# Token tiles' products of one head each, 64 rows by 96 columns, instead of pairs padded with zeros

## The reference

```python
kv = np.einsum('bhsd,bhse->bhde', k, v)          # 8 batches, 8 heads, 576 tokens, 64 dims
out = np.einsum('bhsd,bhde->bhse', q, kv)
rms = np.sqrt(np.mean(out * out, axis=-1, keepdims=True) + 1e-06)
x = out / rms * g_norm                           # to 4608 tokens of 512
logits = x @ phi                                 # 512 x 32 slots
d = softmax of logits over all tokens;  slot_input = d.T @ x
for e in range(8):                               # 4 slots each
    slot_out[e] = np.maximum(slot_input[e] @ w1[e], 0) @ w2[e]   # 512 x 1024, 1024 x 512
c = softmax of logits over slots;  result = c @ slot_out
```

## Time and profile before

| | us |
|---|---|
| median of 3 runs | 171.68 (171.58 to 171.88) |
| the profiled execution | 171.48 |
| its span, first to last instruction | 170.2 |
| TensorE matmuls busy | 148.9 (88%), 1704 records |
| TensorE weight loads busy | 101.0 (59%), 1704 records |
| ScalarE busy | 88.7 (52%) |
| VectorE busy | 87.4 (51%) |
| GpSimd busy | 59.4 (35%) |
| moved by DMA | 71.63 MB in 3555 packets, 421 GB/s |

### The profile page before, as it was taken

One profiled execution on the slowest core, in us unless ns is written; L12 is line 12 of the kernel. 1 busy time (PEld: TensorE's weight loads), 2 busy tenths in 40 slices (PEclk: granted clock), 3 DMA queues, 4 the chain that ended last, 5 costly groups with the idle time before them and its releaser, 6 DMA issues.

```text
span 170.2 us, 3974 instructions
## 1 busy us (share of the span) xinstructions
PE 148.9 (88%) x1704; PEld 101.0 (59%) x1704; DVE 87.4 (51%) x187; ACT 88.7 (52%) x230; POOL 59.4 (35%) x73
## 2 busy tenths in 40 slices
PE   7989889889999899999998999989999789989200
PEld 3468768789688888787985774333436443454000
DVE  1122607672677265765276799634987037218300
ACT  3036758776965887887498882203233045218300
POOL 7000706767256755385716689200000004000000
PEclk9999999999999999999999999999999999999855
DMA  5999999999999999999999899999799999999997
GB/s 184 422 450 421 432 425 478 420 427 470 442 411 409 459 429 431 474 394 446 455 413 485 351 455 434 412 409 485 332 424 443 431 466 383 421 409 439 415 445 306
DMA packets 3555, 71.63 MB, mean 421 GB/s; under 512 B 746, under 2 KB 746, under 8 KB 881
## 3 DMA queue, kind: packets, MB, share of 16 engines
q1 hardware_dynamic: 3137, 71.20, 97.9%
q0 software_dynamic: 400, 0.18, 0.4%
HBM read 61.94 MB, written 9.44 MB: 419 GB/s over the span
## 4 chain that ended last, share of the span: by engine, by line
PE 53%; DMA 24%; ACT 12%; DVE 3%; issue 1%; SPq 1%
PE psum L93 53%; DMA arena<-in_w_dram 14%; DMA arena<-in_kv_dram 9%; ACT bd L93 3%; ACT arena L93 3%; ACT sq L93 2%; ACT part L93 1%; ACT r L93 1%; SPq L93 1%; DVE ms L93 1%; ACT d L93 1%; DVE logits L93 1%; DVE d L93 0%; DVE part L93 0%; DVE arena L93 0%
## 5 line engine op out<-in xcount | busy, mean ns | idle before, releaser
L93 PE MATMUL psum<-bd,arena 128*128 128x192 f32 (+1 forms) x320 | 55.5, 335 | 3.6 <-ACT bd L93 1.4
L93 PEld LDWEIGHTS psum<-bd,arena 128*128 128x128 f32 (+1 forms) x320 | 45.4, 179 | 10.0 <-ACT arena L93 2.8
L93 PE MATMUL psum<-arena 128*64 128x64 f32 (+2 forms) x896 | 36.2, 270 | 1.1 <-DMA arena<-in_w_dram 0.9
L93 PEld LDWEIGHTS psum<-arena 128*64 128x64 f32 (+2 forms) x896 | 27.5, 129 | 13.4 <-issue 5.2
L93 POOL TENSOR_TENSOR part<-part,r 128x512 f32<-128x512 f32 x17 | 17.8, 1048 | 48.8 <-DVE r L93 48.8
L93 POOL TENSOR_TENSOR arena<-arena,r 128x512 f32<-128x512 f32 x34 | 34.7, 1043 | 0.0
L93 ACT COPY arena<-psum 128x512 f32<-128x512 f32 (+2 forms) x48 | 30.7, 649 | 6.0 <-PE psum L93 5.9
L93 DVE TENSOR_REDUCE ms<-sq 128x16 f32<-128x1024 f32 (+1 forms) x19 | 22.1, 1163 | 22.1 <-ACT sq L93 21.6
L93 ACT ACTIVATE sq<-psum 128x512 f32<-128x512 f32 x36 | 21.5, 596 | 10.9 <-PE psum L93 10.6
L93 ACT COPY part<-psum 128x256 f32<-128x256 f32 (+1 forms) x38 | 13.6, 358 | 12.6 <-DVE part L93 11.5
L93 DVE TENSOR_REDUCE logits<-part 128x64 f32<-128x512 f32 (+1 forms) x18 | 17.8, 990 | 0.1
(11 more groups left out here) (77 smaller groups left out, 110.0 us busy)
## 6 DMA issues: line engine op xcount, KB each, us to landing
arena<-in_w_dram SPq DMA_DIRECT2D x2, 8064.0 KB, 29.1
arena<-in_t_dram SPq DMA_DIRECT2D x1, 6912.0 KB, 36.9
arena<-in_w_dram SPq DMA_DIRECT2D x1, 6400.0 KB, 21.6
arena<-in_w_dram SPq DMA_DIRECT2D x3, 2048.0 KB, 17.9
arena<-in_kv_dram SPq DMA_DIRECT2D x2, 2304.0 KB, 19.7
arena<-in_kv_dram SPq DMA_DIRECT2D x1, 4608.0 KB, 42.2
arena<-in_w_dram SPq DMA_DIRECT2D x1, 4096.0 KB, 24.5
arena<-in_kv_dram SPq DMA_DIRECT2D x1, 3584.0 KB, 31.8
```

The costliest lines, as they stand in the source:

```text
L93: self.inst, self.token = method(*args, **kwargs), None
```

## The change

A pair's matmul over 128 rows and 192 columns becomes two matmuls, one for each head, over that head's 64 rows and 96 columns (32 logit columns and 64 of the output). The rows of a head are the half of the partitions on which its dimensions lie, so no zeros are needed and GpSimd sets none. The first heads of the 4 pairs write to one bank, the second heads to another. The middle tiles have four matmuls a pair, 64 rows to 64 tokens. In `Kv.slots` one copy of 128 partitions takes the place of two of 64. The readers of the banks get the order bank, pair, column. `bd_set[0]`, what the first tiles wait for, names all copies of batch 0's last half and the logit columns of its first for all pairs.

```diff
-    bds = [sbuf([P, NPAIR, 192], F32, f"bd{i}") for i in range(2)]
-    bds_zero = []
-    for bd in bds:
-        pool(nc.gpsimd.memset, bd, 0.0)
-        bds_zero.append(pool.done())
+    bds = [sbuf([P, NPAIR, 96], F32, f"bd{i}") for i in range(2)]
...
     def o_bank(T):
-        return shaped(flat(2 * ((T + 1) % 2), 2), [P, NPAIR, 256])
+        two = banks[:, 2 * ((T + 1) % 2) : 2 * ((T + 1) % 2) + 2, : NPAIR * 96]
+        return two.rearrange("p w (j n) -> p w j n", n=96)
...
-            for i in range(2):
-                lo = 64 * i
-                act(
-                    nc.scalar.copy,
-                    self.bd[lo : lo + 64, 2 * a : 2 * z, 32 + lo : 96 + lo],
-                    self.pT[lo : lo + 64, a:z].rearrange("p g (h d) -> p (g h) d", h=2),
-                    after=[bds_zero[self.b % 2], bd_free.get(self.b - 2), turned],
-                )
+            act(
+                nc.scalar.copy,
+                self.bd[:, 2 * a : 2 * z, 32:],
+                self.pT[:, a:z].rearrange("p g (h d) -> p (g h) d", h=2),
+                after=[bd_free.get(self.b - 2), turned],
+            )
...
         for r in range(NPAIR):
-            if t == 4:
...
-            else:
-                i, at = (0, t * P) if t < 4 else (1, (t - 5) * P)
-                pe(
-                    nc.tensor.matmul,
-                    o[:, r, :192],
-                    lhsT=q_main(2 * g + i)[:, r, at : at + P],
-                    rhs=bds[i][:, r],
...
+            for w in range(2):
+                rows = slice(64 * w, 64 * w + 64)
+                if t == 4:
+                    for i in range(2):
+                        pe(
+                            nc.tensor.matmul,
+                            o[64 * i : 64 * i + 64, w, r],
+                            lhsT=q_rest(g)[rows, i, r],
+                            rhs=bds[i][rows, r],
...
+                else:
+                    i, at = (0, t * P) if t < 4 else (1, (t - 5) * P)
+                    pe(
+                        nc.tensor.matmul,
+                        o[:, w, r],
+                        lhsT=q_main(2 * g + i)[rows, r, at : at + P],
+                        rhs=bds[i][rows, r],
...
-            o[:, :, 32:160],
+            o[:, :, :, 32:],
...
-    bd_set[0] = [[halves_set[0][1], halves_set[1][0]], [halves_set[1][1]]]
+    bd_set[0] = [[halves_set[0][1], *halves_set[1]]] * 2
```

More of the change, by code:

```diff
@@ L281, in soft_moe_linear_attention @@
     acc = sbuf([P, 258], F32, "acc")
-    def flat(at, n):
-        return banks[:, at : at + n].rearrange("p b n -> p (b n)")
     def o_bank(T):
-        return shaped(flat(2 * ((T + 1) % 2), 2), [P, NPAIR, 256])
+        two = banks[:, 2 * ((T + 1) % 2) : 2 * ((T + 1) % 2) + 2, : NPAIR * 96]
+        return two.rearrange("p w (j n) -> p w j n", n=96)
     pm = pb = shaped(banks[:, 6], [P, 512])
@@ L370, in slots @@
                 lo = 64 * i
-                dst = self.bd[lo : lo + 64, 2 * a : 2 * z, 160 * i : 160 * i + 32].rearrange("p (g h) n -> p g h n", h=2)
+                dst = self.bd[lo : lo + 64, 2 * a : 2 * z, :32].rearrange("p (g h) n -> p g h n", h=2)
                 src = self.pM[lo : lo + 64, a:z, :, i]
                 if self.b == 0:
-                    dve(nc.vector.tensor_copy, out=dst, in_=src, after=[bds_zero[0], mixed])
+                    dve(nc.vector.tensor_copy, out=dst, in_=src, after=[mixed])
                 else:
@@ L390, in products @@
         for r in range(NPAIR):
-            if t == 4:
-                for i in range(2):
+            for w in range(2):
[7 more added lines that the diff above has]
+                            rhs=bds[i][rows, r],
+                            start=True,
+                            stop=True,
+                            after=[q_landed[g, 1], o_read.get(T - 2), *(second if i else first)[r // 2]],
+                        )
+                else:
+                    i, at = (0, t * P) if t < 4 else (1, (t - 5) * P)
                     pe(
                         nc.tensor.matmul,
-                        o[64 * i : 64 * i + 64, r, :192],
-                        lhsT=q_rest(g)[:, i, r],
-                        rhs=bds[i][:, r],
+                        o[:, w, r],
+                        lhsT=q_main(2 * g + i)[rows, r, at : at + P],
+                        rhs=bds[i][rows, r],
                         start=True,
                         stop=True,
-                        after=[q_landed[g, 1], o_read.get(T - 2), *(second if i else first)[r // 2]],
+                        after=[q_landed[g, int(t > 3)], o_read.get(T - 2), *(second if i else first)[r // 2]],
                     )
-            else:
-                i, at = (0, t * P) if t < 4 else (1, (t - 5) * P)
-                pe(
-                    nc.tensor.matmul,
-                    o[:, r, :192],
-                    lhsT=q_main(2 * g + i)[:, r, at : at + P],
[L408 to L412, removed]
         o_made[T] = pe.done()
@@ L423, in square @@
             nc.scalar.activation,
-            sq[:, T - starts[s]],
-            o[:, :, 32:160],
+            sq[:, T - starts[s]].rearrange("p j (w d) -> p w j d", w=2),
+            o[:, :, :, 32:],
             AF.Square,
@@ L436, in evict @@
         s = stage_of[T]
[L437 to L441, removed]
+        part = part_of(s)[:, T - starts[s]].rearrange("p (j w) n -> p w j n", w=2)
+        act(nc.scalar.copy, part, o[:, :, :, :32], after=[logits_made.get(s - 3), o_made[T]])
+        act(nc.scalar.copy, xts[T % NX][:, :, :128].rearrange("p j (w d) -> p w j d", w=2), o[:, :, :, 32:])
         o_read[T] = part_made[s] = act.done()
@@ L516, in scale_o @@
         s = stage_of[T]
-        r = r_of(s)[:, T - starts[s]].rearrange("p (j w) -> p j w", w=2).unsqueeze(3)
+        r = r_of(s)[:, T - starts[s]].rearrange("p (j w) -> p w j", w=2).unsqueeze(3)
         if of_x:
-            dst = xts[T % NX][:, :, :128].rearrange("p j (w d) -> p j w d", w=2)
-            src = o[:, :, 32:160].rearrange("p j (w d) -> p j w d", w=2)
-        else:
-            dst = part_of(s)[:, T - starts[s]].rearrange("p (j w) n -> p j w n", w=2)
-            src = o[:, :, :192].rearrange("p j (c n) -> p j c n", n=NS)[:, :, 0::5]
+            dst = xts[T % NX][:, :, :128].rearrange("p j (w d) -> p w j d", w=2)
+        else:
+            dst = part_of(s)[:, T - starts[s]].rearrange("p (j w) n -> p w j n", w=2)
+        src = o[:, :, :, 32:] if of_x else o[:, :, :, :32]
         dve(
@@ L527, in scale_o @@
             in0=src,
-            in1=r.to_broadcast([P, 4, 2, D if of_x else NS]),
+            in1=r.to_broadcast([P, 2, 4, D if of_x else NS]),
             op=ALU.mult,
```

## The result

| | before | after |
|---|---|---|
| median, us (20 runs each) | 171.66 (171.49 to 171.97) | 172.11 (171.65 to 174.16) |
| mean granted clock of its runs | 0.969 to 0.979 (its runs beside the experiments) | 0.912 to 0.958 |
| the profiled execution, us | 171.48 | 171.65 |

The ratio is 1.0044 [1.0023, 1.0065]: the changed kernel is slower by 0.44%. Ratios leave out runs over 1.5% above the fastest of their kernel; medians, ranges and counts by clock take in all. 172.11 us is inside the range of the prediction, but not in its likeliest case. The runs also scatter, and the longest were granted the lowest clock: 15 runs at 0.930 to 0.958 took 171.65 to 172.62 us, five at 0.912 to 0.917 took 173.10 to 174.16. The profiled execution is the shortest of the twenty, so its rows show what the change does to the work, and not yet where the time went.

The account below looks back on a forecast made before the run. The DMA queue bounds the kernel: first packets at about 1.7 us, 168.4 of packets, landing at 170.1, execution 1.3 more, median 0.2 above. The change gains nothing at the end: 171.7 us, range 171.2 to 172.6.

Parts of the forecast that it names:

- likeliest case: Whole kernel: time within 0.2% of before, 171.4 to 172.0 us, chance 0.70.
- The bound: SyncE's DMA queue: its 168.4 us of packets set the end, so faster TensorE gains nothing there.
- The products: TensorE's token tiles: row halves run together, 1.04 us a tile; about 16 us less in all.
- The drains: TensorE between unlike shapes: 34 gaps of 0.1 us, 3.4 us at most, leaving a gain of 12.6.
- The loop: Token tile loop: last tile's products 5 to 9 us earlier, with ScalarE and late keys limiting it.
- The program's packets: Instruction fetches by DMA: 640 more TensorE instructions make 2.4 more packets, 0.84 us each on one engine.
- rival (a): DMA engines that end last take the added instruction packets: 172.5 us with one, 173.4 with two; chance 0.14.
- The range: Whole kernel: 171.2 to 172.6 us, leaving out some 0.15 of the chances.
- rival (b): TensorE idles before the weights landing at 124.7 and its clock drops, losing about 2.4 us; chance 0.05.
- a margin of 2.6: Last store's issue: 2.6 us of slack before its lateness would delay the end.
- two cold waits: Both TensorE waits for weights cold, nothing taken back: 2 x 1.8 - 2.6 = 1.0 us, giving 172.7.
- 5.5 us at the 6,400 KB load: That load's issue: slack before the queue runs dry, for the engine that ends last.

Follow-up runs that it names:

- lean_before: Kernel before, loading only the first 8,064 KB of weights, which all experts use, results kept elsewhere: 168.65 us, ratio 0.9825.
- warm_late: Changed kernel plus ten matmuls on zeros before the products that wait for the 6,400 KB load: 172.00 us, ratio 1.0036 against the kernel before.
- before_waits: Kernel before, plus 18 always-met waits behind each of 34 token tiles: 171.71 us, ratio 0.9998.
- warm_all: Changed kernel plus matmuls on zeros at tiles 9, 24, 31, 33 and the 6,400 KB load's wait: 171.92 us, ratio 1.0011 against the kernel before.
- after_again: The changed kernel unaltered, run again on another chip: 172.21 us, ratio 1.0030 against the kernel before.

## Why the prediction came out as it did

**The bound.** Right: the queue moves 71.20 MB in 97.9% and 97.8% of all engines' time, before and after. It missed how close the second bound is: `lean_before` puts the chain of instructions at 3.0 us below it, and in the long execution of `warm_late` that chain set the end.

**The products.** Right in the mechanism, nearly in size: 8 pairs of records in 1.14 us from start to end instead of 1.04. The products of all tiles are busy 41.1 us, before 55.8: 14.7 of the 16 expected. TensorE as a whole gained 9.3 us of the 12.6. Two groups with records at the low clock are busy 3.1 us more (1.6 in the experts' first products, 1.5 in the products of keys and values).

**The drains.** 0.1 us each, as taken from the earlier trace rows. The weight loads around the last broadcast of the sums, after and then before:

```profile
96.55 0.97 PEld L93 LDWEIGHTS psum<-bd,arena 64*128 64x128 f32 x16 [0.42 <-issue]
97.62 0.30 PEld L93 LDWEIGHTS psum<-diag,ones 128*128 128x128 f32 x2
97.95 0.97 PEld L93 LDWEIGHTS psum<-bd,arena 64*128 64x128 f32 x16
```

```profile
98.50 1.27 PEld L93 LDWEIGHTS psum<-bd,arena 128*128 128x128 f32 x8 [0.42 <-ACT sq L93]
99.75 0.35 PEld L93 LDWEIGHTS psum<-diag,ones 128*128 128x128 f32 x2
100.02 1.28 PEld L93 LDWEIGHTS psum<-bd,arena 128*128 128x128 f32 x8
```

After, the broadcast's loads begin 0.10 us behind the end of the tile's, before 0.02 ahead of it; from there to the next tile's loads it is 0.33 us, before 0.27. That is 0.2 more for two changes of shape. By the Trainium skill (TensorEngine Tiling (Array Packing), Key Properties) a change of the tiling mode drains TensorE; the trace agrees.

**The loop.** The direction was right, the size wrong: 2.1 us shorter, not 5 to 9. I had said that keys not yet landed would hold some of it back; they hold much of it, 2.68 us at tile 9 and 1.81 at tile 24, since a loop that gets ahead meets the same landing times. Behind 85 us the chain that ended last goes through the softmax steps of VectorE and ScalarE, which the change leaves as they were. The 6,400 KB load was issued at 101.14, not before 99.

**The program's packets.** 16, as foreseen. One more costs nothing (`before_waits`); three cost at most what `warm_all` keeps, 0.11% [0.03, 0.20], unless something else there gains, and were not isolated. In the form of rival (a), a packet on an engine that ends last, they are not the cause of the long executions, since `warm_all` has 16 too. The prediction missed that TensorE itself can stand still at such a packet.

**The range.** 172.11 us lies in it, but the likeliest case, no change, did not come, and the upper end was set by one packet of rival (a). That the range held is luck.

**The step that failed** is rival (b), to which I gave 0.05. "TensorE cools" is what happens, but the step placed it at one wait, the one for the load landed at 124.7, priced it at 2.4 us and set it against a margin of 2.6. Its sum for two cold waits then took 1.8 us for each, a term that no row gives. Three things in it were wrong. The place: that wait does cool TensorE (5.26 us for 3.64), and filling it took about 0.25 us off the common executions, but the long ones stayed. They need a fall in the loop, ahead of an issue. The size: a fall of almost 14 us, after a stretch in which TensorE was busy 2.98 us of 5 and its longest wait was 1.21 us; the prediction looked for long idling alone. And the margins: 5.5 us at the 6,400 KB load was read off the engine that ends last, with the remark that others may run out earlier. With the issue 2.4 us later than in the earlier trace rows the rate over the next 15 us was 408 GB/s instead of 432, at a margin that still read 3.1. What is lost so is not made good, because the queue has no spare rate.

**What stays open.** Why the same program draws a clock of 0.95 in one execution and 0.917 in the next, with the same 1.20 us wait at 91 us; why packets took longer from 145 to 150 us in the long one; and the remaining 0.1% at a held clock: three packets, TensorE's gaps at them, or loads that are issued 1 to 2 us earlier and interleave differently with others. The way from the low clock to the late end is read from two long executions only. No version that moves all weights beat the kernel before.

## What to carry to other kernels

Where transfers are the bound, time saved on TensorE turns into waits, and waits can cost clock: before speeding up an engine with slack, list the waits it will meet, and which issue stands behind each. Do not count on the whole margin of an issue that is read off the slowest engine, ask how far the chain of instructions is behind the transfers, and time such a change over a dozen runs beside their granted clocks, since one profile can show either kind of execution.

## What the runs showed of the hardware

- A low clock can come without a long wait and stay under full load: in `after_again` TensorE was busy 2.98 us of 5 with waits up to 1.21, then 13.7 us at 0.50 with TensorE busy all the time. The short execution of the same program, busy 2.92 of 5 with the same wait, kept 1.00. The Trainium skill (TensorE: Matmul & The Clock Gate, A second HAM failure mode: psum-queue depth-cycling) has a kernel whose short idles between groups of matmuls cost it the clock; the trace of `after_again` agrees.
- TensorE can stand still at a packet of instructions: ten gaps of 0.24 to 2.67 us in six kept executions, each ending 2.2 to 2.5 us after such a packet began.
- A wait that is already met is free up to a point: 18 behind each of 34 tiles cost nothing, 48 cost 25.7 us.
- Weight loads of 128 columns on two halves of the rows run in pairs: a tile's 16 loads take 0.97 us (at 96.55), 0.12 us a pair, where one load alone repeated each 0.13.
